# Reordered steps in a fused attention, dense expert layer and routed expert layer, with one weight split moved from VectorE to GpSimd

## What is computed

```
x = attention(q, k, v)                      # 2304 tokens x 512
h = x @ w_in                                # 512 -> 1024
solu = h * softmax(h)
ln = (solu - mean(solu)) / sqrt(var(solu) + 1e-6) * g_ln
x = ln @ w_out                              # 1024 -> 512
logits = (x/|x|) @ (emb/|emb|).T / tau      # 8 experts
e = argmax(logits);  gate = softmax(logits)[e]
out = gate * (relu(x @ w1[e]) @ w2[e])
```

## Time and profile before

| | us |
|---|---|
| median of 3 executions (1182.45 to 1183.18) | 1182.48 |
| the profiled execution | 1183.76 |
| its span | 1181.9 |
| PE busy in the span | 1119.8 |
| DVE, ACT, POOL busy | 765.9, 628.6, 471.8 |
| mean granted TensorE clock, share of full | 0.966 |

### The profile page before, as it was taken

The page is one execution under the profiler, slowest core; times in us unless marked ns, Lnnn a source line. Parts: engine busy times, 40 slices in busy tenths (PEclk is TensorE's granted clock), DMA queues, the critical chain, the costliest instruction groups (busy, mean ns, idle before and its releaser), DMA issues.

```text
span 1181.9 us, 20776 instructions
## 1 busy us (share of the span) xinstructions
PE 1119.8 (95%) x6615; PEld 877.4 (74%) x6615; DVE 765.9 (65%) x1965; ACT 628.6 (53%) x1344; POOL 471.8 (40%) x478
## 2 busy tenths in 40 slices
PE   7899999999999999999898999997589999999996
PEld 6777777777777777776576888885468878888885
DVE  6687777777777777786557898896834551414110
ACT  5566666667666666665363544344335652525221
POOL 6666556666565666633333341232011111211111
PEclk8699999999999999999998999997789999999999
DMA  4211122221111222010420000023545571511100
GB/s 133 64 45 41 42 62 61 61 62 42 58 41 43 61 62 61 21 58 35 144 81 19 21 25 19 27 76 121 163 167 170 185 249 37 189 37 37 47 28 1
DMA packets 55843, 85.60 MB, mean 72 GB/s; under 512 B 10094, under 2 KB 28526, under 8 KB 55600
## 3 DMA queue, kind: packets, MB, share of 16 engines
q1 hardware_dynamic: 51728, 72.91, 19.4%
q0 software_dynamic: 4000, 11.28, 3.0%
HBM read 74.73 MB, written 11.27 MB: 73 GB/s over the span
## 4 chain that ended last, share of the span: by engine, by line
PE 42%; DVE 4%; issue 2%; POOL 1%; ACT 1%; DVEq 0%; ACTq 0%; POOLq 0%
PE h_ps L773 9%; PE h_ps L775 8%; PE h_ps L774 8%; PE o_ps L773 4%; PE o_ps L775 4%; PE o_ps L774 4%; PE t_ps L1271 2%; PE t_ps L1163 1%; DVE junk L1342 1%; PE h_ps L1238 1%; POOL emb L1098 1%; DVE w_split L1590 1%; PE h_ps L1286 0%; ACT junk_sq L1640 0%; DVE w_split L1560 0%
## 5 line engine op out<-in xcount | busy, mean ns | idle before, releaser
L569 DVE TENSOR_REDUCE maxes<-s_ps 128x1 f32<-128x384 f32 x432 | 226.7, 548 | 37.2 <-PE s_ps L416 26.8
L329 POOL TENSOR_SCALAR probs<-probs,recips 128x1152 f32<-128x1152 f32 x128 | 157.7, 1232 | 163.8 <-DVE recips L586 163.8
L416 PE MATMUL s_ps<-kq 128*128 128x384 f32 x768 | 202.1, 374 | 7.9 <-ACT probs L733 5.8
L595 DVE COPY pt<-even_ps 128x384 f32<-128x384 f32 x279 | 155.4, 557 | 77.8 <-PE even_ps L455 77.7
L489 PE MATMUL pv_ps<-pt,values 128*64 128x320 f32 (+1 forms) x1152 | 171.5, 418 | 1.2 <-DVE pt L595 0.7
L1079 POOL DMA_INDIRECT out<-junk,target_rows x25 | 25.8, 1031 | 286.2 <-ACT junk L1763 286.2
L702 ACT COPY pt<-odd_ps 128x384 f32<-128x384 f32 x144 | 69.0, 479 | 133.0 <-PE odd_ps L455 133.0
L416 PEld LDWEIGHTS s_ps<-kq 128*128 128x128 f32 x768 | 127.3, 197 | 9.5 <-ACT probs L733 6.1
L455 PE MATMUL even_ps<-ident,probs 128*128 128x128 f32 x693 | 130.2, 286 | 1.5 <-DVE pt L595 1.4
L455 PEld LDWEIGHTS even_ps<-ident,probs 128*128 128x128 f32 x693 | 81.9, 142 | 60.7 <-issue 51.2
L489 PEld LDWEIGHTS pv_ps<-pt,values 128*64 128x64 f32 x1152 | 70.4, 136 | 72.5 <-issue 35.7
(11 more groups left out here) (290 smaller groups left out, 2381.7 us busy)
## 6 DMA issues: line engine op xcount, KB each, us to landing
w_raw_e<-in_moe_w SPq DMA_DIRECT2D x60, 512.0 KB, 5.4
k_raw<-in_k SPq DMA_DIRECT2D x32, 288.0 KB, 2.9
values<-in_v SPq DMA_DIRECT2D x16, 576.0 KB, 3.9
token_rows<-x_rows SPq DMA_DIRECT2D x18, 256.0 KB, 2.0
q_raw<-in_q SPq DMA_DIRECT2D x32, 128.0 KB, 3.0
q_raw<-in_q SPq DMA_DIRECT2D x16, 256.0 KB, 3.0
w_raw<-in_moe_w_in SPq DMA_DIRECT2D x4, 512.0 KB, 5.9
w_raw<-in_moe_w_out SPq DMA_DIRECT2D x4, 512.0 KB, 4.0
```

The lines of the kernel that those rows point to most:

```text
L329: nc.gpsimd.tensor_scalar(part, part, recips[:, par, s:s + 1], 1.0, ALU.mult, ALU.mult).then_inc(norm_done, 1)
L416: last = nc.tensor.matmul(bank[:, 0:chunk], left, right, start=(i == 0), stop=(i == len(parts) - 1))
L569: nc.vector.tensor_reduce(maxes[:, e, c:c + 1], bank, AX.X, ALU.max).then_inc(max_done, 1)
L595: nc.vector.tensor_copy(pt[(par + s) % 2][:, i * 3 * P:(i + 1) * 3 * P], bank[:, 0:3 * P]).then_inc(t_out[i], 1)
```

## The change

Line numbers of the new file differ. In words:

- GpSimd no longer multiplies the embeddings; the dot products take the factor as a scalar per partition. The refinement of that factor moves one step later, and on ScalarE the squares, logarithm and exponential for it stand at the end of steps 1 and 2.
- VectorE's dot products run in portions (`dots_due`): two before `solu_of`, the others after both `low_y`; nine a step in steps 4 to 11, then eight. `find_spots(0, 12)` stands at the end of step 16.
- At the seam ScalarE makes expert 0's high parts ahead of `rows(last)`; VectorE's four low parts are spread out (`low_first`).
- In the expert layer `relu(0)`, `high_x(1)` and `high_h(0)` come before all that waits for the gates; `weigh` (the gate chain) goes into step 1, its matmuls into step 2. `place_of` stands behind `turn_h`. `down_e` waits for the low half that it needs, twice. GpSimd makes the four low parts of expert 1's first matrix, ahead of the fourth gather.

```diff
 (GpSimd)
-                if at == 2:
-                    pool.wait_ge(emb_factor_ready, 1)
-                    for e in range(experts):
-                        nc.gpsimd.tensor_scalar(emb[:, e, :], emb[:, e, :], emb_stat[:, 3, e:e + 1], 1.0, ALU.mult,
-                                                ALU.mult).then_inc(emb_scaled, 1)
...
             gather(2)
+            for c in range(part):
+                pool.wait_ge(w1_hi_done, c + 1)
+                lo, hi = slot_at(0, 1, c), slot_at(0, 0, c)
+                nc.gpsimd.tensor_tensor(w_split[:, lo:lo + chunk], w_raw[:, c, :],
+                                        w_split[:, hi:hi + chunk].bitcast(F32), ALU.subtract).then_inc(w1_lo_done, 1)
 (TensorE)
-                pe.wait_ge(h_lo_done, halves * (t + 1))
...
                 for f in range(ff_blocks):
+                    if f % (ff_blocks // 2) == 0:
+                        pe.wait_ge(h_lo_done, halves * t + f // (ff_blocks // 2) + 1)
...
+                if t >= 1:
+                    turn_h(t - 1)
                 if t == 1:
                     pe.wait_ge(tiles_known, 1)
                 if 1 <= t < slot_tiles:
                     now = place_of(t)
-                if t >= 1:
-                    turn_h(t - 1)
...
-                if t >= 1:
-                    down_e(t - 1, *gone)
-                if t == 1:
+                if t == 2:
                     pe.wait_ge(factors_picked, 1)
...
+                if t >= 1:
+                    down_e(t - 1, *gone)
 (VectorE)
+                        out=junk[:, e % 2, :], in0=x_rows[:, m % ring, :], scalar=emb_stat[:, 3, e:e + 1],
+                        in1=emb[:, e, :], op0=ALU.mult, op1=ALU.mult, accum_out=lg[:, m, e:e + 1]).then_inc(dots_done, 1)
...
+                return max(0, min((experts + 1) * (at - emb_lag), experts * (at - 2)))
...
+                maximum(at)
+                due = dots_due(at - 1)
+                dots(due, min(due + 2, dots_due(at)))
+                solu_of(at)
+                if at >= 1:
                     for half in range(2):
                         low_y(at - 1, half)
+                dots(min(due + 2, dots_due(at)), dots_due(at))
...
+            low_x(1)
+            low_h(0)
+            low_first(3)
+            for t in range(1, slot_tiles):
+                split_next(t, 0, w1_hi_done, w1_lo_done)
+                if t + 1 < slot_tiles:
+                    low_x(t + 1)
+                if t == 1:
+                    weigh()
+                low_h(t)
+                if t == 1:
                     dve.wait_ge(factors_done, 1)
...
+                    split_next(0, part, w2_hi_done, w2_lo_done)
                 split_next(t, part, w2_hi_done, w2_lo_done)
 (ScalarE)
             high_x(0)
+            relu(0)
+            high_x(1)
+            high_h(0)
+            split_next(0, 0, w1_hi_done, up_e_done, 0)
             act.wait_ge(tiles_known, 1)
+            for t in range(1, slot_tiles):
+                split_next(t, 0, w1_hi_done, up_e_done, halves * t)
+                relu(t)
                 if t + 1 < slot_tiles:
                     high_x(t + 1)
+                if t == 1:
+                    act.wait_ge(shifted, 1)
+                    nc.scalar.activation(work[:], work[:], ACT.Exp).then_inc(exped, 1)
+                if t == 2:
+                    act.wait_ge(factors_ready, 1)
+                    scale(0)
+                if t >= 2:
+                    scale(t - 1)
+                high_h(t)
+                if t == 1:
+                    split_next(0, part, w2_hi_done, down_e_done, 0)
+                split_next(t, part, w2_hi_done, down_e_done, t)
```

220 lines of the change are left out of this document (104 added, 116 removed).

## The result

| | before | after |
|---|---|---|
| median, us | 1182.47 (1181.38 to 1183.18, 4 runs) | 1172.40 (1171.72 to 1173.10, 4 runs) |
| span of the profiled execution | 1181.9 | 1170.0 |
| PE, DVE, POOL busy | 1119.8, 765.9, 471.8 | 1114.8, 784.9, 478.9 |
| mean granted TensorE clock | 0.966 | 0.979 |

A forecast was written before the change was run, and what follows sets the result against it. TensorE was taken to bound the dense layer's steady steps, so only its waits elsewhere could be won: -8.2 + 2.6 + 0 - 15.6 - 0.6 = -21.8 us, from 1182.5 to 1160.7 us; range 1153 to 1170 us.

The forecast's parts named there:

- Part 1: Start of the dense layer: the 5.88 us wait at `up(4)` and its restart go; 8.2 us gained.
- Part 2: Dense layer's steady steps: nothing gained or lost; VectorE's 1.3 us of added work fits its 1.45 us idle.
- part 5: First steps of the expert layer: earlier `relu(0)` and low parts shorten TensorE's waits; 15.6 us gained.
- VectorE becomes the bound of the dense layer: Rival: wait for `low_y`'s second half doesn't shrink when VectorE is late, 27 us lost: 1188 us; chance 0.03.
- Part 3: End of the dense layer: 3.3 us wait shrinks, 4 us wait for GpSimd's centring at `turn(17)` comes; 2.6 us lost.
- Part 4: Seam between dense and expert layer: `turn_rows(1)` starts as before; 0 us, bounds 0 and +1.5.
- Parts 5 and 6: Expert layer's first steps, 15.6 us gained, and its tail, where `down_e(24)` starts sooner, 0.6 us gained.
- Register loads: Rival: loads behind short transposes come out in each of 24 expert steps; 1161 to 1169, about 1166 us; chance 0.24.
- Longer blocking in the expert layer: Rival: GpSimd and VectorE block each other longer, `up_e(2)` waits 3 us; +4 to +6, 1166 us; chance 0.10.
- the change doesn't do what it says: Rival: first expert steps stay bound by something hidden, most of part 5 given back; 1172 us; chance 0.05.

The follow-up runs named there:

- dots_first: Changed kernel with all dots of each dense-layer step ahead of `solu_of` and `low_y` again, ninth dot and factor kept; 1164.6 us, 0.9841 of before.
- spots_first: Changed kernel with step 16's search for the spots ahead of the last six dots and their `route`; 1171.8 us, 0.9907 of before.
- hybrid: Changed kernel with all dots ahead of `solu_of` up to step 11, and step 16's search ahead of the last six dots; 1162.6 us, 0.9825 of before.
- no_factor: Changed kernel with dots times constant 1.0 instead of the factor in memory, eight a step and never nine; 1166.0 us, 0.9860 of before.
- low_on_vector: Changed kernel with the four low parts of expert 1's first matrix made by VectorE again, not GpSimd; 1172.0 us, 0.9908 of before.

## Why the prediction was wrong

**Part 1 was right**: -8.3 us for -8.2. No wait at `up(4)`, and the steps there are 12.06 us long.

**Part 2 is the step that failed**: "the steady steps: nothing", and 10.9 us were lost there. It failed at two terms, and the experiments have a price for each: 5.3 us for the room, 5.6 for the order.

First, the room. "VectorE idles 1.45 us in a step" was read from one row of one step, and the sum "1.3 us, it just fits" was held against it for all steps. The added work itself was sized near enough, 1.3 us for a measured 0.61 + 0.42 = 1.03 in the period. But in four steps GpSimd splits a matrix beside the dots. Before the change that already lengthened the dots by 0.7 us in step 6, rising to 2.0 in step 9 (1.62 and 1.75 us for two dots of 0.69), so that its period without the added work is up to 12.5 us. dots_first, which has the work but not the new order, is 5.3 us longer than the kernel before in the steady steps.

Second, the order. Part 2 saw in the moved dots only `low_y`'s wait for the second half (it came: 2.52 us once, in step 4, and 0.48 to 0.49 us in steps 5 to 8). It did not ask which instructions of VectorE GpSimd's now run beside. GpSimd's centring is released by `solu_of`, and the weight and x splits follow it. Before, `low_y` and `maximum` filled that time, which read PSUM and were not held up. Now dots come right behind `low_y`: the dot beside the weight takes 2.46 us in place of 1.63, and the wait of 0.48 us comes on top: 1.3 of the 1.42 us a step. And x's low part, which met no dot outside these four steps before, now holds one for 1.02 us in every step from 4 on but step 9, where it holds an instruction of `route`; in steps 10 and 11, with nine dots, TensorE's step is 12.71 and 12.74 us long for it. The prediction used this very mechanism with its row in part 5, and not in part 2.

The dot of 2.46 us in the row at 660.60 is in keeping with the Trainium skill (SBUF — State Buffer, section SBUF: two separate sides), by which the one that comes second blocks fully until the other's instruction ends: GpSimd's weight split ends at 662.52, and the dot 0.54 us later.

**The rival "VectorE becomes the bound of the dense layer"** (0.03) is what happened in steps 4 to 11, by another route than it gave. Its point of decision, 12.1 us, was right; its mechanism (a wait for `low_y` that doesn't shrink) was not, and it was priced for all steps.

**Part 3 had the sum about right for a wrong reason.** It wanted a wait of 4 us ahead of `turn(17)`, released by GpSimd; measured were 5.78 us ahead of `down(16, 0)`, released by VectorE. The failing term is "`y_lo` is there at about 799.7": it counted two dots ahead of `low_y` but left out that VectorE enters the step 6.9 us late, with six dots and the search of the step before still ahead, and with what part 2 had lost: 6.32 us of wait in spots_first are 2.37 in hybrid. With the wait for VectorE that long the search's place doesn't matter. Its own mechanism, the late centring, shows in no_factor with 2.60 us. That 3.2 us measured lie near the 2.6 forecast is luck.

**Part 4 was right** (+0.7, bounds 0 and 1.5). **Parts 5 and 6 were right**: -16.5 us for -16.2. `up_e(1)` came 8.4 us after `up_e(0)` (7.8 forecast), no wait at `up_e(2)`, 3.64 us at `up_e(3)` (4.0), with a restart of 2.7 us (15.17 us from `up_e(3)` to `up_e(4)`, where 12.50 is the rule; 2.4 forecast). The last `down_e` waits 1.31 us for 1.86. Within part 5, blocking by GpSimd was charged with up to 1.2 us; the chain was blocked, but in the changed kernel TensorE waited only 0.16 us for it, and in low_on_vector, without the block, the expert layer is 0.3 us shorter.

**The other rivals.** Register loads: steps of 12.49 to 12.50 us but for one of 14.36, with a wait for a weight split that the kernel before has too (1.59 us in both), and the last, of 12.07; no idle time without a releaser; refuted. Longer blocking in the expert layer: the four low parts took 10.38 us, as the forecast had them (9.5 + 1), and `up_e(2)` did not wait; refuted. The price of "the change doesn't do what it says", 1172 us, is the time measured, but by chance: part 5 came in full. The range ended at 1170 for want of part 2's terms.

## What to carry to other kernels

Room on an engine is read in the fullest step, and separately for each kind of step: one idle row of one step says nothing about a neighbour in which another engine has extra work. When instructions with two SBUF inputs are moved on VectorE, look at what GpSimd does at their new place, and at what their old neighbours, which read PSUM, had been covering. In a loop of stages "behind the last instruction of the step" means "ahead of the first of the next", and that shows at the last step, when nothing covers it any more. An engine that has fallen behind and has a period as long as the loop's carries its lateness to that point.
